# Sinks' value product of an attention stage in one rounded pass, with V's sink rows made on TensorE

## What is computed

```python
# attention: B, H, S, D = 4, 8, 768, 64; n_sink, window = 4, 128
keep = is_sink | in_window            # first 4 keys, or the last 128
a = softmax(where(keep, scale * q @ k.T, -1e9))
x = (a @ v)                           # rows of 512 = H * D
# experts: w_gate 512 x 8
logits = x @ w_gate + modality_bias[modality_id]
e_idx = argmax(logits)
x = gate_w * (relu(x @ w1[e_idx]) @ w2[e_idx])
# feed-forward
h = x @ w_in
out = (h / (1 + exp(-1.702 * h))) @ w_out
```

## Time and profile before

| | |
|---|---|
| median of 3 executions | 1104.45 us (1104.09 to 1106.42) |
| profiled execution | 1103.77 us |
| its span, first to last instruction | 1102.0 us |
| TensorE busy | 1090.4 us, 99% of the span |
| weight loads | 932.3 us |
| VectorE, ScalarE, GpSimd busy | 434.9, 385.5, 347.3 us |
| line 973 (sinks' value product) | 64 records, mean 435 ns |
| line 968 (value products) | 704 records, mean 270 ns |

### The profile page before, as it was taken

One profiled execution on the slowest core, in us unless ns is written; L12 is line 12 of the kernel. 1 busy time (PEld: TensorE's weight loads), 2 busy tenths in 40 slices (PEclk: granted clock), 3 DMA queues, 4 the chain that ended last, 5 costly groups with the idle time before them and its releaser, 6 DMA issues.

```text
span 1102.0 us, 18596 instructions
## 1 busy us (share of the span) xinstructions
PE 1090.4 (99%) x5883; PEld 932.3 (85%) x5884; DVE 434.9 (39%) x1112; ACT 385.5 (35%) x798; POOL 347.3 (32%) x484
## 2 busy tenths in 40 slices
PE   9999999999999999999999999999999999999998
PEld 9999999988888888888888888888888888888887
DVE  5666666679321234122364223222323222222222
ACT  3666667754222133222353222222222222222222
POOL 8899999852466212121120001001001001000100
PEclk9999999999999999999999999999999999999999
DMA  9998899415731133121041001001000001000101
GB/s 217 234 257 202 226 233 245 128 49 181 265 126 38 57 106 132 38 84 40 29 181 58 20 1 48 20 8 42 25 10 38 19 19 38 0 0 0 39 1 39
DMA packets 59700, 96.27 MB, mean 87 GB/s; under 512 B 8192, under 2 KB 33024, under 8 KB 59648
## 3 DMA queue, kind: packets, MB, share of 16 engines
q1 hardware_dynamic: 53888, 76.75, 25.0%
q0 software_dynamic: 5760, 18.89, 5.0%
HBM read 76.21 MB, written 19.41 MB: 87 GB/s over the span
## 4 chain that ended last, share of the span: by engine, by line
PE 94%; DVE 2%; issue 2%; ACT 2%; DVEq 0%; POOL 0%; ACTq 0%; POOLq 0%
PE psum L1264 8%; PE psum L1262 8%; PE psum L1263 8%; PE psum L1255 8%; PE psum L1254 8%; PE psum L1253 8%; PE psum L968 5%; PE psum L1193 4%; PE psum L1162 4%; PE psum L1199 4%; PE psum L1196 4%; PE psum L1166 4%; PE psum L1170 4%; PE psum L943 3%; PE psum L1181 2%; PE psum L931 2%
## 5 line engine op out<-in xcount | busy, mean ns | idle before, releaser
L2048 DVE TENSOR_TENSOR g<-psum,g 128x512 f32<-128x512 f32 x96 | 66.3, 691 | 292.2 <-ACT g L1483 292.2
L1483 ACT ACTIVATE g<-psum 128x512 f32<-128x512 f32 x96 | 57.3, 598 | 305.4 <-PE psum L1255 304.6
L1262 PE MATMUL psum<-w_hi,gT_hi 128*128 128x512 f32 x384 | 151.4, 394 | 0.0
L900 POOL DMA_INDIRECT out<-o_out,out_rows x20 | 21.5, 1074 | 409.3 <-ACT o_out L1503 404.7
L1264 PE MATMUL psum<-w_hi,gT_lo 128*128 128x512 f32 x384 | 149.6, 390 | 0.0
L1263 PE MATMUL psum<-w_lo,gT_hi 128*128 128x512 f32 x384 | 149.6, 390 | 0.0
L1255 PE MATMUL psum<-x2T,win_lo 128*128 (+1 forms) x384 | 149.6, 389 | 0.0
L1253 PE MATMUL psum<-x2T,win_hi 128*128 (+1 forms) x384 | 149.6, 389 | 0.0
L1254 PE MATMUL psum<-x2T,win_hi 128*128 (+1 forms) x384 | 149.4, 389 | 0.0
L968 PE MATMUL psum<-v_sb,pT 128*128 128x73 f32 x704 | 106.2, 270 | 3.2 <-DVE pT L1773 1.6
L1761 DVE CUSTOM_DVE_ANT_0 s_msk<-psum,mask_sb 128x260 f32<-128x260 f32 (+1 forms) x192 | 75.1, 403 | 68.8 <-PE psum L932 37.6
(11 more groups left out here) (313 smaller groups left out, 1884.9 us busy)
## 6 DMA issues: line engine op xcount, KB each, us to landing
qk_raw<-qkT SPq DMA_DIRECT2D x64, 384.0 KB, 7.5
stage<-w SPq DMA_DIRECT2D x12, 1024.0 KB, 7.0
x<-y_rows SPq DMA_DIRECT2D x24, 256.5 KB, 2.6
vT_sb<-vT SPq DMA_DIRECT2D x16, 384.0 KB, 5.1
v_sb<-vP SPq DMA_DIRECT2D x16, 384.0 KB
x_rows<-x_sb SPq DMA_DIRECT2D x16, 384.0 KB, 3.3
win_raw<-w SPq DMA_DIRECT2D x16, 256.0 KB, 4.3
win_raw<-w_in SPq DMA_DIRECT2D x16, 256.0 KB, 5.3
```

Source lines behind the costliest of these rows:

```text
L1262: pe.matmul(psum[:, OB[t], :], gh, hi, start=(f == 0), stop=False)
L2048: dve.tensor_tensor(g32[:, f % 2, :], psum[:, FB[f % 2], :], g32[:, f % 2, :], ALU.mult)\
```

## The change

- `p_sinks` gets groups of 32 rows for each of the four tiles; each group holds the tile's sink probabilities three times (KINDS = 3; `pack_sinks` broadcasts). After the transpose VectorE makes from them, per row, a rounded value or the rest of it: a rounded copy `pT_sinks_hi` ahead of `pT`, and behind `pT` a scalar-tensor-tensor operation with a 0/1 column `kinds` into `pT_sinks` (fp32r).
- `v_sinks` (fp32r, one pair at a time instead of four) holds in these three groups of rows the high or the low part of V and gates, so that the three terms of the split product are summed along the contraction of one rounded matmul.
- V's sink rows come from TensorE: `sink_w` holds the two heads' gate columns with a 128-column identity between them (144 columns), and line 992's product with `vT_sinks` yields gates and V rows on all partitions. `split_sinks` rounds and splits them in steps 5, 6 and 7 of a pair.
- The sink loads (line 439) and `sink_pick` are gone. VEXT is 74 (was 73), LW 16 (was 64).
- q and k come from the host with the sink keys already in place, so `split_qk` and `split_first` have four operations, not six.
- `iota`s and constants are made by GpSimd between heads; `add_heads` moves from step 4 to step 6 of the next batch; the ranks of the early tile go from step 29 to 33, the early ranks from 43 to 46; the indices of the early tiles are taken from PSUM.

```diff
-    EXP_AT, RANK_AT_STEP = 38, 43
+    EXP_AT, RANK_AT_STEP = 38, 46
-    OPEN_RANK_STEP, OPEN_INV_STEP = 29, 16
+    OPEN_RANK_STEP, OPEN_INV_STEP = 33, 16
-    LW, VW = 64, 80
-    VEXT = D + 1 + E
+    LW, VW = 16, 80
+    VEXT = D + 2 + E
+    GROUP, KINDS = 32, 3
+    SINK_W = P + 2 * E
...
-                for t in range(SINK_T):
-                    sp.dma_start(v_sinks[t * SINKS:(t + 1) * SINKS, c, t, both],
-                                 vP[b, c, 0:SINKS, 0])\
-                      .then_inc(v_loaded[c], 16)
...
             def split_qk(r, slot):
...
                 pool.tensor_copy(q_st[:, slot, :], raw_q).then_inc(qk_rounded, 1)
-                pool.tensor_copy(hi[:, :, 0:P], blocks_k).then_inc(qk_rounded, 1)
-                pool.tensor_copy(hi[:, :, P:SEG], sinks_k).then_inc(qk_rounded, 1)
+                pool.tensor_copy(k_hi[:, slot, :], raw_k).then_inc(qk_rounded, 1)
...
+            between = {2: make_iotas, 5: make_consts, 9: make_biases, 11: open_logits, 12: open_ties, 13: open_chain, 16: open_choice,
...
             def turn_probs(b, n):
...
+                if (n - 2) % QT == QT - 1 and b * H + n >= QT:
+                    pe.wait_ge(sinks_turned, b * H + ((n - 2) // QT + 1))
...
             def weigh_values(b, n):
...
+                    pe.wait_ge(sinks_split, SINK_T * (b * PAIRS + c + 1))
+                    pe.wait_ge(sinks_turned, b * H + h + 1)
                     mm = pe.matmul(psum[:, O_ps[h % 2], FIRST_S * VW:QT * VW]
                                    .rearrange("p (t n) -> p t n", n=VW)[:, :, 0:VEXT], pT_sinks[:],
-                                   v_sinks[:, c, :, half * VEXT:(half + 1) * VEXT],
+                                   v_sinks[:, :, half * VEXT:(half + 1) * VEXT],
                                    start=False, stop=True, skip_group_check=True)
...
             def weigh_gates(b, c, part):
...
                     pe.wait_ge(sinks_spread, g + 1)
-                    pe.matmul(psum[0:COPIES * SINKS, VW_ps, QT * LW:(QT + 1) * LW], vT_sinks[:, g % 2, :],
-                              wg_sb[:, c, :], start=True, stop=True).then_inc(vw_ready, 1)
+                    pe.wait_ge(sink_w_ready, 1)
+                    pe.matmul(psum[:, VW_ps, SINK_AT:SINK_AT + SINK_W], vT_sinks[:, g % 2, :],
+                              sink_w[:, c, :], start=True, stop=True).then_inc(vw_ready, 1)
...
             def move_probs(b, n):
...
+                turned = psum[:, PT_ps[n % 2], BAND:BAND + P]
                 if n % QT == QT - 1 and SINK_T:
-                    dve.tensor_copy(pT_sinks[:], psum[:, PT_ps[n % 2], BAND:BAND + P])
+                    dve.tensor_copy(pT_sinks_hi[:], turned).then_inc(sinks_high, 1)
                 dve.tensor_copy(pT[:, n % 2, 0:w], psum[:, PT_ps[n % 2], 0:w]).then_inc(pT_moved_dve, 1)
+                if n % QT == QT - 1 and SINK_T:
+                    dve.wait_ge(sinks_high, b * H + n // QT + 1)
+                    dve.scalar_tensor_tensor(out=pT_sinks[:], in0=turned, scalar=kinds[:, 1:2],
+                                             in1=pT_sinks_hi[:].bitcast(F32), op0=ALU.mult, op1=ALU.subtract)\
+                       .then_inc(sinks_turned, 1)
...
+            def split_sinks(b, c, k):
+
+                own = psum[:, VW_ps, SINK_AT:SINK_AT + SINK_W]
+                if k == 0:
+                    then(dve.tensor_scalar(v_sinks_hi[:], own, signs[:, 0:1], None, ALU.mult))
+                for t in ((0,), (1,), (2, 3))[k]:
+                    rows = slice(t * GROUP, (t + 1) * GROUP)
+                    dve.scalar_tensor_tensor(out=v_sinks[rows, t, 2:2 + SINK_W], in0=own[rows], scalar=signs[rows, 1:2],
+                                             in1=v_sinks_hi[rows].bitcast(F32), op0=ALU.mult, op1=ALU.add)\
+                       .then_inc(sinks_split, 1)
...
             def step(b, n):
                 if n < HT:
                     mask_scores(b, n)
+                if n < HT and 0 <= n % (2 * QT) - SINK_STEP < 3:
+                    split_sinks(b, n // (2 * QT), n % (2 * QT) - SINK_STEP)
...
-                if n == HT + PV_LAG and b < B - 1:
-                    add_heads(b, H)
+                if b and n == PV_LAG + 2:
+                    add_heads(b - 1, H)
                     dve.sem_inc(logits_added, 1)
-                if b == 0:
-                    make_consts(n)
...
-                if n == 45:
+                if n == HT:
                     take_ranks(pre, psum[:, VW_ps, 0:PRE * E].rearrange("p (t e) -> p t e", e=E), 1)
```

More of the change, by code:

```diff
@@ L103, in program @@
     MASKS = 3
-    assert BAND + P <= BANK and SINK_ROWS <= P
+    assert BAND + P <= BANK
     dve_takes = [i == QT - 1 for i in range(QT)]
@@ L682, in make_biases, with make_consts @@
                         then(pool.tensor_tensor(bias_of[:], bias_of[:], biases[:], ALU.add))
+            def make_consts():
+                pool.tensor_copy(tri[:], tri_f[:]).then_inc(consts_copied, 1)
+                pool.tensor_copy(ones[:], ones_f[:]).then_inc(consts_copied, 1)
+                pool.tensor_scalar(from_end[:], iota_row[:, 0:E], -1.0, float(E), ALU.mult, ALU.add)\
+                    .then_inc(consts_copied, 1)
+                then(pool.memset(lower[:], 1.0))
+                pool.affine_select(out=lower[:], in_=lower[:], compare_op=ALU.is_gt, fill=0.0, base=0,
+                                   pattern=[[1, E], [-1, E]], channel_multiplier=0).then_inc(consts_copied, 1)
+                pool.wait_ge(consts_copied, 4)
             def open_logits():
@@ L738, in open_rows @@
                 then(pool.tensor_scalar(open_scatter[:], open_valid[:], iota_dump[:, 0:1], None, ALU.add))
+                then(pool.tensor_scalar(seen[:, QT:PRE:QT, :], row(from_end[:], [P, B - 2, E]), 0.0, None, ALU.mult))
             def split_open(j):
@@ L1663, in rows_in_tile @@
                                                 in1=rank_cnt[:, tiles], op0=ALU.mult, op1=ALU.add)
-            def make_consts(n):
-                if n == 36:
-                    dve.tensor_copy(tri[:], tri_f[:])
-                if n == 37:
-                    dve.tensor_copy(ones[:], ones_f[:]).then_inc(consts_copied, 1)
-                if n == 38:
-                    then(dve.tensor_scalar(from_end[:], iota_row[:, 0:E], -1.0, float(E), ALU.mult, ALU.add))
             def choose_open(n):
```

207 lines of the change are left out of this document (105 added, 102 removed).

## The result

The changed kernel takes 1123.56 us (median of 6 runs, 1115.0 to 1132.0) against 1104.82 us (1104.09 to 1107.67) before: a ratio of 1.014, 95% interval 1.0096 to 1.0185. It is slower, by 1.4%. The forecast was 1095.0 us, faster. The profiled execution took 1123.74 us with a span of 1121.6, at a mean granted clock of 0.986.

The account below looks back on a forecast made before the run. TensorE's stream was taken to bound the attention, with pT from VectorE as its late input; -12.0 + 0.5 + 6.3 - 1.9 - 1.7 - 0.6 = -9.4 us took 1104.45 to 1095.0 us, range 1089.0 to 1100.5.

Parts of the forecast that it names:

- The sinks' product: TensorE's value product of the sinks (line 973): rounded, it saves 0.375 us each, 32 times, -12.0 us.
- the +0.5 us: TensorE's product of V's sink columns (line 992), widened from 64 to 144 columns: 0.25 instead of 0.21 us, 16 times.
- the first rival: VectorE's new work is hidden whole, so its +6.3 falls to about 0: 1089 us, chance 0.14.
- VectorE's new work: Split operations in steps 5 to 7 of a pair delay pT for TensorE: +6.3 us, ends +1.5 and +12.
- The cover: VectorE's idle time and closer masks before the sinks' copy leave it 0.21 us late from 1.2 us new work.
- The worse pairs: Other VectorE work in step 6: +0.73 at three batch starts, +1.2 in batch 3's last pair; +0.6 in batch 1's last.
- What leaves VectorE: from_end and lower go to GpSimd, with casts and index reads also changed, between masks: -1.9 us.
- the ranks: Early ranks (line 1002) at step 46 instead of 43, covering TensorE's 1.67 us idle wait for GpSimd: -1.7 us.
- the start: VectorE's first split loses two operations of 24 columns, and small copies leave the first mask's way: -0.6 us.
- GpSimd: It loses two 24-column operations per head and makes constants, some 4 us, in gaps between heads: put at nothing.
- the third: VectorE becomes the bound in steps 5 to 9, all 1.6 us a pair on TensorE's path: 1114 us, chance 0.07.
- The last rival: The rounded sinks' product takes 0.50 us like the old one: sum +2.6, 1107 us, chance 0.04.

Follow-up runs that it names:

- e1: The changed kernel with the split of V's sink rows made for the first pair only: 1096.6 us, ratio 0.992 to the kernel before.
- e15: The changed kernel with two of the split's four block operations (both of step 7) left out for all pairs but the first: 1097.5 us, ratio 0.994.
- e6: The kernel before with only the add of a finished batch's heads moved from step 4 to step 6: 1104.1 us, ratio 0.999.
- e3: The changed kernel with VectorE's moved single steps (add of heads, early gates, open expert's choice) put behind step 9: 1107.3 us, ratio 1.002.
- e19: The changed kernel, moved single steps put late, with all four block operations of the split on the first 32 partitions: 1099.0 us, ratio 0.994.
- e13: The changed kernel, moved single steps put late, with immediate numbers for the [P,1] scalars of the split's five operations: 1104.1 us, ratio 0.998.
- e5: The changed kernel, moved single steps put late; one dense VectorE operation makes all sink rows, ScalarE places four blocks: 1099.4 us, ratio 0.994.
- e8: e5 with two of the four blocks placed by VectorE copies from SBUF in step 7 instead of by ScalarE: 1152.2 us, ratio 1.044.
- e2: The kernel before plus five VectorE operations like the new split's, in steps 5 to 7 of 13 of the 16 pairs: 1128.5 us, ratio 1.021.
- e16: e5 with the copy of pT put ahead of the sinks' rounded copy in every head's last step: 1098.3 us, ratio 0.993.

## Why the prediction was wrong

- *What bounds the kernel, and where it would be late*: right. TensorE's stream sets the end, and the wait that grew is the one for `pT` in step 9.
- *The sinks' product, -12.0 us*: nearly right. It takes 0.11 us of the stream, for 0.125. Together with the +0.5 us the prediction had 0.72 us less a pair, and an ordinary pair without the split is 13.48 - 12.84 = 0.64 us shorter (e1). For the whole kernel the sum without the split was -15.7 us, the first rival's 1089, and e1 came to -9. If the sum's other terms held, e1's wait of 2.4 us and its 7 us at half the clock (some 3.4 us lost) make most of the 7 us between them.
- *VectorE's new work, +6.3 us*: the step that failed. It priced the lateness at 0.21 us in an ordinary pair, and it is 1.09 (the wait of 0.35 us has become 1.44). The price of 0.215 us an operation was taken from a copy of 128 columns at partition 0, which lets its successor overlap it. Measured against the prediction's stretch: the rounded product 0.40 for 0.335, the first block 0.28 for 0.215, the second 0.10 + 0.40 for 0.215, the last two 0.11 + 0.81 for 0.43. That is 0.065 + 0.065 + 0.285 + 0.49 = 0.90 us, the whole difference between 2.48 and 3.37. The upper bound of 0.3 us for an operation was too low; the range's end of +12 us rested on it.
- *The cover*: right. The prediction hid 1.0 us of its 1.2. Of the 2.10 us that the new work takes in steps 5 to 7 1.0 is hidden, and of the 1.18 us in e15 again 1.0.
- *The worse pairs, 0.73, 1.2 and 0.6 us*: right places, wrong sizes. The move of the add costs nothing by itself (e6), but on top of the late split it has its full 1.2 us. With its fellows it makes 16 us, about 11 of them by the clock, which the prediction left at 1.00. That is the second thing that it put at nothing without a reason.
- *What leaves VectorE, the ranks, the start, GpSimd*: not tested alone. TensorE's 1.67 us of idle time before the ranks isn't there after, where TensorE comes 22 us later, and not in e15 either, where it comes 2 us earlier than in the kernel before (226.93 against 229.20 us).
- *How the miss of 28.6 us adds up*, as an estimate from these readings: 0.88 us too little lateness in 16 pairs, 14 us; the single steps with the clock, 16 us for some 3; the product, 1 us.
- *The rivals*: the third was the right mechanism at a chance of 0.07, with its own test in it ("the new operations at twice 0.215 us", "over 0.75 us later"): they came to 1.9 times at the most and to 1.1 us. But it reckoned with no cover, which is there, and its 1114 us lies above what lateness alone makes (e3, 1107) and below the result, since it had no clock in it. The last rival is out: the product takes 0.11 us.
- *Small slips in the sums*, none of which changes the outcome: 0.04 us for the wider product of line 992, 16 times, is +0.6 and not +0.5; the range's end with VectorE's bill at +12 is 1100.7 and not 1100.5; the chances of the forecast and the first rival add up to 0.81 and not 0.82.

## What to carry to other kernels

Price an operation by its distance from start to start in the queue where it will stand, and on the partitions where it will work; where no such row exists, the upper end should be its full duration plus a gap on both sides. Slack hides the first operations almost whole and none of the last, so add up a stretch with the highest price before calling it hidden. Where several single steps can fall into the same late stretch, look at the granted clock too: here five waits cost more in the clock than in themselves, and not in every execution.

## What the hardware showed

- A VectorE operation of 32x144 that starts at other partitions than its neighbours starts 0.10 us later behind the read ahead of it and takes 0.40 us to the next start, against 0 and 0.28 us at the same partitions (changed kernel and e19).
- A [P,1] operand instead of an immediate costs 60 ns of 365 (e13); 32 or 128 partitions make no difference (365 and 362 ns, the changed kernel and e5).
- A 32x144 copy from SBUF to SBUF on VectorE takes 226 ns alone and up to 1906 beside GpSimd's operations (e8).
- After waits of 1.6 to 2.6 us TensorE's clock was at 1.2 GHz for 3 to 17 us, though not after each of them: in the profiled execution of e3, with waits of up to 1.7 us, it stayed at 2.4 GHz all through the attention, and so it did after 2.25 us in e2. In e16 it was low for 3 to 4 us with no such wait ahead of it.
